# Placing four table columns in the route and the others in the layer's head, in a kernel of linear attention and two expert layers

## The chip, the cores and the metric

The kernel runs on one core of one Trainium2 chip. The metric is the device time of the whole program in microseconds. An execution of the kernel before takes 586.45 us in the median of three (585.61 to 586.54). One more was profiled; the times of the trace are microseconds from the start of its span.

## What is computed

Attention writes 3072 rows of 384 numbers. Each of two expert layers then finds the best of 8 experts for every row, and multiplies the row by that expert's two weight matrices (384 x 1024 and 1024 x 384). In the first layer a row is left alone where its skip score is not positive; in the second every row is replaced.

```python
def _moe_ref(x, w_skip, w_gate, w1, w2) -> np.ndarray:
    ...
    logits = xc @ w_gate
    e_idx = np.argmax(logits, axis=1)
    ...
    gate_w = probs[np.arange(len(xc)), e_idx]
    y = np.zeros_like(xc)
    for e in range(E):
        mask = e_idx == e
        ...
        h = np.maximum(xc[mask] @ w1[e], 0.0)
        y[mask] = gate_w[mask, None] * (h @ w2[e])
    out[do_compute] = xc + y
```

## The kernel before

Three blocks run one after another for each layer's boundary: `attention`, then for each layer m (0 and 1; layer one and layer two in the text) `route` and `moe`. Each is a block of five engine programs with its own semaphores, and between blocks all engines meet at a barrier. Inside a block each engine goes through its own queue in the order in which it is written.

`route` sorts the 3072 rows (24 chunks of 128, `TILES`) by expert. In layer two it first loads the rows back, turns them on PE, copies them out on ACT and DVE (`x_out`, L567) and computes the logits. In both layers DVE then runs a chain of some twenty small operations: best expert, softmax sum (`den`, whose reciprocal is the gate), ranks, and for each row a slot of a table. The slot has a row of the table (`row_i`, slot mod 128) and a column (`col_i`, slot / 128). The table has 128 rows and 38 columns in layer one, 45 in layer two (`NCOL`); column t holds the row ids, and the gates, of the 128 rows that tile t of the expert work takes.

The table is filled on PE. For each chunk, `row_hot` (128 x 128, is the slot's row equal to this one) is the stationary side, and `col_hot` (128 x 2 NCOL: one-hot column times the id, one-hot column times the gate) the moving side; 24 products add up in PSUM (L688). They are float32 products; each stands in the trace as two instructions. DVE makes the column comparison (L781), the gates' half (L784) and `row_hot` (L572, eight operations); ACT makes the ids' half (L721, 24 operations). At the end DVE copies the sums into `table` (L802, L803). Between these stand pieces of another job: the weights of the first expert are split into a high part (`w_hi`, ACT, L856) and a low part (`w_lo`, DVE, L861), fourteen pieces of each, six for w1 and eight for w2. `stay_warm` (L22) runs transposes on PE that nobody reads.

`moe` begins with a head: Pool gathers the first rows (two tiles in layer one, four in layer two) by the table's first columns (L1038), PE turns them (`turn_x`, L1115), ACT rounds them to the high part (`x_high`, L1203), DVE subtracts for the low part (`x_low`, L1252). In the head PE first runs four transposes (L1121) and 24 warm-up transposes (L22). Then come the experts, in units of tiles: `up` (L1132 to L1134, eight column blocks k, each of nine float32r products; block k >= 4 waits for `h_lo` of block k - 4, made by ACT and DVE, L1220, L1221, L1292), then `down` with the second matrix, whose results DVE multiplies by the gate (L1269) and Pool scatters (L1059). While a unit runs, ACT and DVE split the next expert's weights. At the end of layer one SP waits for the last scatter and loads the rows for layer two's route (`load_rows`, L455, L457), in groups of 512 rows.

In layer two's route the programs of ACT and DVE stand inside a loop of one turn whose first instruction is put at the start of a line of instructions (`from_line_start`, `head_slot` 0), so that entering it is a jump.

## Time and profile before

| | us |
|---|---|
| median of three executions | 586.45 |
| the profiled execution, whole | 586.31 |
| its span (first to last instruction) | 584.3 |
| PE busy, matmul | 545.2 |
| DVE busy | 381.5 |
| ACT busy | 262.8 |
| Pool busy | 250.0 |

The mean granted clock of PE over the span is 0.977 of full speed. A reader should look at where layers begin. Attention ends at about 133, layer one's route runs from 133 to 151 and its experts from 160 to 290. Layer two's rows are loaded from 296, its route ends at 337, and its experts run from 347 to 577. Since PE is nearly always busy in between, the timeline of the short stretches around the two routes says more than the page's totals.

### The profile page before, as it was taken

How to read it: one execution, taken by the hardware profiler on the slowest of the kernel's cores; microseconds unless marked ns; L12 is line 12 of the kernel's file. 1: busy time of each engine (PE TensorE's matmuls, PEld its weight loads, DVE VectorE, ACT ScalarE, POOL GpSimd, SP SyncE). 2: the span in 40 equal slices, each digit the busy share in tenths (PEclk: the TensorE clock that was granted, in tenths of full speed). 3: DMA queues.
4: the chain of work that ended last, by engine and by line, in shares of the span. 5: the costliest groups of instructions: out<-in, count | busy, mean ns of one | idle time of the engine just before them, and what ended most of it. 6: DMA issues, size and time to landing. Idle time of an engine off the chain costs nothing. (4 is left out here: it accounts for less than half of the span.)

```text
span 584.3 us, 16263 instructions
## 1 busy us (share of the span) xinstructions
PE 545.2 (93%) x5606; PEld 517.6 (89%) x5607; DVE 381.5 (65%) x832; ACT 262.8 (45%) x752; POOL 250.0 (43%) x356
## 2 busy tenths in 40 slices
PE   4899999988699999999969869999999999999994
PEld 4799999978699999999967859999999999999994
DVE  5789888958598888888704917463747463637341
ACT  1233333325477667776504416262737361627230
POOL 5987778732244444555410042232424322425241
PEclk9999999997799999999999989999999999999998
DMA  9788888776287777776378023544354444111101
GB/s 156 135 166 176 163 165 164 153 257 218 56 304 228 214 222 252 243 235 209 65 249 308 1 61 97 196 139 168 116 191 154 158 140 154 50 42 46 41 2 39
DMA packets 114145, 89.59 MB, mean 153 GB/s; under 512 B 80689, under 2 KB 104948, under 8 KB 114097
## 3 DMA queue, kind: packets, MB, share of 16 engines
q1 hardware_dynamic: 105760, 73.96, 44.6%
q0 software_dynamic: 7776, 14.82, 9.2%
q8 instruction: 26, 0.43, 0.3%
q10 hardware_dynamic: 560, 0.20, 0.2%
q14 instruction: 23, 0.18, 0.1%
HBM read 80.44 MB, written 13.27 MB: 160 GB/s over the span
## 5 line engine op out<-in xcount | busy, mean ns | idle before, releaser
L861 DVE TENSOR_TENSOR w_lo<-w_raw,w_hi 128x384 fp32r<-128x384 f32 (+1 forms) x224 | 130.1, 607 | 5.6 <-ACT w_hi L856 3.4
L1132 PE MATMUL e_ps_h<-e_x_hi,w_hi 128*128 128x192 f32 (+3 forms) x384 | 120.8, 315 | 2.6 <-DVE e_x_lo L1252 2.6
L856 ACT CAST w_hi<-w_raw 128x384 fp32r<-128x384 f32 (+1 forms) x224 | 120.0, 566 | 4.0 <-issue 4.0
L1133 PE MATMUL e_ps_h<-e_x_lo,w_hi 128*128 128x192 f32 (+3 forms) x384 | 120.6, 314 | 0.0
L1134 PE MATMUL e_ps_h<-e_x_hi,w_lo 128*128 128x192 f32 (+3 forms) x384 | 120.5, 314 | 0.0
L1292 DVE SCALAR_TENSOR_TENSOR e_h_lo<-e_ps_h,e_h_hi 128x128 fp32r<-128x128 f32 (+1 forms) x192 | 70.2, 395 | 46.6 <-ACT e_h_hi L1221 43.1
L1132 PE MATMUL e_ps_y<-w_hi,e_h_hi 128*128 128x384 f32 x272 | 95.5, 351 | 0.0
L1134 PE MATMUL e_ps_y<-w_hi,e_h_lo 128*128 128x384 f32 x272 | 91.5, 336 | 0.0
L1133 PE MATMUL e_ps_y<-w_lo,e_h_hi 128*128 128x384 f32 x272 | 91.1, 335 | 0.0
L1132 PEld LDWEIGHTS e_ps_h<-e_x_hi,w_hi 128*128 128x128 f32 x384 | 73.7, 192 | 4.9 <-DVE e_x_lo L1252 3.1
L1133 PEld LDWEIGHTS e_ps_h<-e_x_lo,w_hi 128*128 128x128 f32 x384 | 73.7, 192 | 1.3
L1134 PEld LDWEIGHTS e_ps_h<-e_x_hi,w_lo 128*128 128x128 f32 x384 | 73.6, 192 | 1.3
L1220 ACT ACTIVATE e_h_lo<-e_ps_h 128x64 fp32r<-128x64 f32 x128 | 29.3, 229 | 79.1 <-PE e_ps_h L1134 76.0
L1221 ACT ACTIVATE e_h_hi<-e_ps_h 128x256 fp32r<-128x256 f32 (+1 forms) x128 | 59.4, 464 | 0.0
L1252 DVE TENSOR_TENSOR e_x_lo<-e_ps_x,e_x_hi 128x384 fp32r<-128x384 f32 (+1 forms) x54 | 28.2, 523 | 45.0 <-ACT e_x_hi L1203 44.7
L1133 PEld LDWEIGHTS e_ps_y<-w_lo,e_h_hi 128*128 128x128 f32 x272 | 51.3, 189 | 0.1
L1132 PEld LDWEIGHTS e_ps_y<-w_hi,e_h_hi 128*128 128x128 f32 x272 | 51.2, 188 | 0.1
L1134 PEld LDWEIGHTS e_ps_y<-w_hi,e_h_lo 128*128 128x128 f32 x272 | 51.0, 188 | 0.0
L1203 ACT CAST e_x_hi<-e_ps_x 128x384 fp32r<-128x384 f32 (+1 forms) x54 | 24.5, 456 | 54.8 <-PE e_ps_x L1115 54.8
L1047 POOL DMA_INDIRECT x_in<-x_rows,e_ent_in x33 | 37.5, 1138 | 26.8 <-POOL e_ent_in L1043 26.8
L1059 POOL DMA_INDIRECT out_dram<-y_rows,e_ent_out x19 | 18.5, 973 | 62.7 <-DVE y_rows L1269 54.6
L224 ACT COPY xT<-ps_x 128x384 f32<-128x384 f32 x24 | 11.5, 480 | 71.4 <-PE ps_x L368 71.4
(170 smaller groups left out, 932.8 us busy)
## 6 DMA issues: line engine op xcount, KB each, us to landing
w_raw<-in_moe_w_dram SPq DMA_DIRECT2D x32, 1536.0 KB, 7.0
r_in<-in_r_dram SPq DMA_DIRECT2D x24, 192.0 KB, 3.2
k_in<-in_k_dram SPq DMA_DIRECT2D x24, 192.0 KB, 4.1
v_in<-in_v_dram SPq DMA_DIRECT2D x24, 192.0 KB, 4.0
x_rows<-rows SPq DMA_DIRECT2D x24, 192.0 KB, 3.4
w_lo<-x_rows SPq DMA_DIRECT2D x5, 768.0 KB, 9.4
w_lo<-x_rows SPq DMA_DIRECT2D x2, 384.0 KB, 3.6
x_in<-x_rows,e_ent_in POOLq DMA_INDIRECT x33, 3.1
```

Of the source, the lines that this page charges most:

```text
L856: act.copy(self._of(self.hi1[par], self.hi2[par], n), self._of(self.raw1[par], self.raw2[par], n)).then_inc(self.hi_done[par], 1)
L861: eng.tensor_tensor(self._of(self.lo1[par], self.lo2[par], n), self._of(self.raw1[par], self.raw2[par], n), self._of(self.hi1[par], self.h ...
L1047: pool.indirect_dma_start(x_in[n][:], None, rows, bass.IndirectOffsetOnAxis(ap=ent_in[n][:, 0:1], axis=0), bounds_check=bound, oob_is_err= ...
L1059: pool.indirect_dma_start(out_rows, bass.IndirectOffsetOnAxis(ap=ent_out[slot][0:count, 0:1], axis=0), y_rows[slot][0:count, :], None, bou ...
L1132: pe.matmul(o, s_hi, m_hi, start=(k == 0), stop=False)
L1133: pe.matmul(o, s_hi, m_lo, start=False, stop=False)
L1134: return pe.matmul(o, s_lo, m_hi, start=False, stop=(k == last))
L1203: act.copy(x_hi[:, :, w], ps_x[n % 2][:, 0:D].rearrange("p (c t) -> p c t", c=DC)[:, :, 0:w.stop - w.start]).then_inc(x_hi_done, 1)
L1220: act.activation(h_lo[:, k, top_at:top_at + HALF], ps_h[k % 4][:, TOP], ACT.Relu).then_inc(h_top_done, 1)
L1221: act.activation(h_hi[:, k, :], ps_h[k % 4][:, 0:XW], ACT.Relu).then_inc(h_hi_done, 1)
L1252: dve.tensor_tensor(x_lo[:, :, w], ps_x[n % 2][:, 0:D].rearrange("p (c t) -> p c t", c=DC)[:, :, 0:w.stop - w.start], x_hi[:, :, w].bitcas ...
L1292: ins = dve.scalar_tensor_tensor(h_lo[:, k, lo_at[n]:lo_at[n] + of.stop - of.start], ps_h[k % 4][:, of], 0.0, h_hi[:, k, of].bitcast(F32), ...
```

## The change

In the route only four columns of the table (`AHEAD`) are placed, ids only. The id is split into the number of its 128 rows (`chunk_of`) and its place in them (`part_of`), both small whole numbers, so that float32r products, in one pass, hold them exactly; DVE puts them together. `row_hot` is float32r. Comparisons for all columns, the gates' half (DVE), the ids' half (ACT, twelve operations for the first twelve chunks, DVE for the others) and the 24 float32 products of all columns move into the head of `moe`, on all engines there, with the turns of the first rows between the products. DVE then waits for all 24 (`rest_placed`) and copies the rest of the table and the gates; in layer one eight of the fourteen w_lo pieces come after this. Before, six came after the last `x_low`. The head's 24 warm-up transposes go. ACT has all fourteen w_hi pieces of layer one in the route. The loop that begins a line is taken off ACT's and DVE's programs in layer two's route; a loop of one turn with one register move, at the start of a line, is put at the end of their programs in layer one's `moe`.

```diff
-NOWHERE = 1 << 20
+NOWHERE = 32 * P
+AHEAD = 4
...
+            pool.iota(ids[:], order, base=-NOWHERE, channel_multiplier=1, **exact).then_inc(id_made, 1)
+            pool.iota(chunk_of[:], [[step // P, count] for step, count in order], base=-NOWHERE // P, channel_multiplier=0, **exact).then_inc(id_made, 1)
+            pool.iota(part_of[:], [[0, 1]], base=0, channel_multiplier=1, **exact).then_inc(id_made, 1)
...
             for n in range(PLACES):
-                if n % (PLACES // 2) == 0:
-                    pe.wait_ge(gates_placed, 2 * n // PLACES + 1)
-                pe.wait_ge(ids_placed, n + 1)
+                if n == 0:
+                    pe.wait_ge(few_ready, 2)
                 pe.wait_ge(rows_ready, n + 1)
                 for q in range(GP):
                     i = GP * n + q
-                    ins = pe.matmul(ps_placed, row_hot[:, i, :], placing[:, 2 * NCOL * i:2 * NCOL * (i + 1)], start=(i == 0), stop=(i == TILES - 1))
+                    ins = pe.matmul(ps_few, row_hot[:, i, :], few_hot[:, i, :], start=(i == 0), stop=(i == TILES - 1))
...
-            with from_line_start(act):
...
-                    for n in range(W.N1):
-                        W.hi(act, 0, 0, n)
-                act.wait_ge(id_made, 1)
-                for place in range(PLACES):
...
-                        ins = act.mul(col_hot[:, i, 0, :], col_is[:, i, :], entry[:, i, 0:1])
-                    ins.then_inc(ids_placed, 1)
-                if not TURN:
-                    for n in range(W.N1, W.N):
-                        W.hi(act, 0, 0, n)
+            if not TURN:
+                for n in range(W.N):
+                    W.hi(act, 0, 0, n)
...
-                for n in range(2):
...
-                    dve.tensor_tensor(col_is[:, i, :], row_iota[:, 0:NCOL].unsqueeze(1).to_broadcast(wide),
-                                      col_i[:, i].unsqueeze(2).to_broadcast(wide), ALU.is_equal).then_inc(col_equal, 1)
...
-                    dve.tensor_tensor(col_hot[:, i, 1, :], col_is[:, i, :], entry[:, i, 1].unsqueeze(2).to_broadcast(wide), ALU.mult).then_inc(gates_placed, 1)
...
+            few = [P, TILES, AHEAD]
+            link(dve.tensor_tensor(few_is[:], row_iota[:, 0:AHEAD].unsqueeze(1).to_broadcast(few), col_i[:].unsqueeze(2).to_broadcast(few), ALU.is_equal))
+            dve.wait_ge(id_made, 3)
+            dve.tensor_tensor(few_hot[:, :, 0:AHEAD], few_is[:], chunk_of[:].unsqueeze(2).to_broadcast(few), ALU.mult).then_inc(few_ready, 1)
+            dve.tensor_scalar(few_hot[:, :, AHEAD:2 * AHEAD], few_is[:], part_of[:], None, ALU.mult).then_inc(few_ready, 1)
...
+            link(dve.tensor_scalar(few_at[:], ps_few[:, 0:AHEAD], float(P), float(NOWHERE), ALU.mult, ALU.add))
+            dve.tensor_tensor(table[:, 0:AHEAD], few_at[:], ps_few[:, AHEAD:2 * AHEAD], ALU.add)
...
+        def fetch_next_line(eng):
+
+            reached = eng.alloc_register(f"{tag}_reached")
+            with nc.Fori(0, 1, engines=[eng.engine], head_slot={eng.engine: 0}) as _:
+                eng.reg_mov(reached, 1)
...
+            pool.wait_ge(rest_out, 2)
...
-            stay_warm(pe, ident, ps_y[0][:, 0:P], 3)
-            for n in range(X):
-                turn_x(0, n)
+
+
+            def place(i):
+
+                if i < PART:
+                    pe.wait_ge(gates_hot, 1)
+                    pe.wait_ge(ids_hot, i // 3 + 1)
+                else:
+                    pe.wait_ge(rest_hot, 6)
+                pe.matmul(ps_y[1][:, 0:2 * USED], row_hot[:, i, :].bitcast(F32), hot_of(i), start=(i == 0), stop=(i == TILES - 1)).then_inc(rest_placed, 1)
+            ahead = [PART, PART + 2, PART + 6, PART + 10] if m else [PART, PART + 4]
+            for i in range(TILES):
+                if i in ahead:
+                    turn_x(0, ahead.index(i))
+                place(i)
...
+            act.wait_ge(col_equal, 1)
+            for i in range(PART):
+                ins = act.mul(col_hot[0][:, i, 0, :], is_col[:, i, :].bitcast(F32), ids[:, i:i + 1])
...
+            for n in range(2):
+                i = slice(PART * n, PART * n + PART)
+                wide = [P, PART, USED]
+                dve.tensor_tensor(is_col[:, i, :], row_iota[:, 0:USED].unsqueeze(1).to_broadcast(wide), col_i[:, i].unsqueeze(2).to_broadcast(wide), ALU.is_equal).then_inc(col_equal, 1)
...
+            dve.wait_ge(col_equal, 2)
+            hot(0, 1, gate).then_inc(gates_hot, 1)
+            for n in range(1, 4):
+                hot(n, 0, ids).then_inc(rest_hot, 1)
+                hot(n, 1, gate).then_inc(rest_hot, 1)
...
-                for n in range(W.N1 // 2, W.N1 + 2):
+                for n in range(W.N1 // 2, W.N1):
                     W.lo(dve, 0, 0, n)
             for n in range(X):
                 x_low(0, n)
+            dve.wait_ge(rest_placed, TILES)
+            dve.tensor_scalar(table[:, AHEAD:USED], ps_y[1][:, AHEAD:USED], float(NOWHERE), None, ALU.add).then_inc(rest_out, 1)
+            dve.tensor_copy(gates[:, 0:USED], ps_y[1][:, USED:2 * USED]).then_inc(rest_out, 1)
             if m == 0:
-                for n in range(W.N1 + 2, W.N):
+                for n in range(W.N1, W.N):
                     W.lo(dve, 0, 0, n)
...
             run_experts(dve, expert)
+            if m == 0:
+                fetch_next_line(dve)
```

## Rows read from the trace of the kernel before

**Rows 1.** Busy us by window and engine; then PEclk, DMA share, GB/s

```profile
151.10:157.70 6.60, 4.97 (x24) 5.00 (x25) 2.83 (x5) 0.16 (x1) 2.74 (x2) 0.50 0.15 44
...
160.40:289.80 129.40, 129.39 (x959) 126.92 (x960) 108.91 (x283) 90.64 (x262) 61.21 (x68) 1.00 0.70 223
...
304.70:307.90 3.20, 3.13 (x20) 2.78 (x24) 1.33 (x4) 0.96 (x2) 0.00 (x0) 0.50 1.03 368
...
345.70:352.30 6.60, 5.31 (x17) 5.28 (x17) 1.58 (x3) 1.48 (x4) 2.68 (x5) 0.50 0.16 40
```

**Rows 2.** Timeline of layer one's route: start, us, engine, line, operation, [idle before]

```profile
141.49 0.64 DVE L781 TENSOR_TENSOR m_col_is<-m_row_iota,m_col_i 128x456 f32<-128x456 int32 x1
...
142.23 2.72 ACT L721 ACTIVATE m_placing<-m_col_is,m_entry 128x38 f32<-128x38 f32 x12 [4.49 <-DVE m_col_is L781]
...
142.71 1.96 DVE L572 TENSOR_TENSOR m_row_hot<-m_row_iota,m_row_i 128x384 f32<-128x384 int32 x4
...
143.90 5.48 PE L688 MATMUL m_ps_places<-m_placing,m_row_hot 128*128 128x76 f32 x48
...
147.67 1.89 DVE L861 TENSOR_TENSOR w_lo<-w_raw,w_hi 128x512 fp32r<-128x512 f32 x3
...
147.87 3.39 ACT L856 CAST w_hi<-w_raw 128x384 fp32r<-128x384 f32 x8
...
149.48 0.25 DVE L791 TENSOR_TENSOR m_over_short<-m_seen,m_short_limit 128x96 f32<-128x96 f32 x1
...
150.34 0.19 DVE L802 TENSOR_SCALAR table<-m_ps_places 128x38 int32<-128x38 f32 x1
```

**Rows 3.** Timeline of layer one's head and first unit

```profile
152.73 2.83 DVE L861 TENSOR_TENSOR w_lo<-w_raw,w_hi 128x512 fp32r<-128x512 f32 x5 [2.10 <-issue]
...
153.61 4.84 PE L22 MATMUL e_ps_y<-ident 128*128 128x128 f32 x24
...
154.01 1.52 POOL L1038 DMA_INDIRECT x_in<-x_rows,table  x1 [0.30 <-issue]
...
160.27 2.91 DVE L861 TENSOR_TENSOR w_lo<-w_raw,w_hi 128x384 fp32r<-128x384 f32 x6
...
160.41 0.36 PE L1132 MATMUL e_ps_h<-e_x_hi,w_hi 128*128 128x192 f32 x1 [1.30 <-DVE e_x_lo L1252]
...
163.10 0.48 DVE L1292 SCALAR_TENSOR_TENSOR e_h_lo<-e_ps_h,e_h_hi 128x128 fp32r<-128x128 f32 x2
...
168.58 0.36 PE L1132 MATMUL e_ps_y<-w_hi,e_h_hi 128*128 128x384 f32 x1
```

**Rows 4.** Timeline as layer two begins; landing of the load issued in 296.8:297.3

```profile
303.76 0.86 ACT L567 COPY m_xT<-m_ps_xT 128x384 f32<-128x384 f32 x2 [17.16 <-issue]
...
304.77 2.82 PE L644 MATMUL m_ps_xT<-ident,w_lo 128*128 128x128 f32 x12 [3.56 <-DMA w_lo<-x_rows]
...
w_lo<-x_rows SPq DMA_DIRECT2D x1, 768.0 KB, 7.8
```

**Rows 5.** Timeline of layer two's route and head

```profile
328.13 0.72 DVE L781 TENSOR_TENSOR m_col_is<-m_row_iota,m_col_i 128x540 f32<-128x540 int32 x1
...
334.65 0.35 DVE L795 TENSOR_TENSOR m_over<-m_over,m_of_full 128x192 f32<-128x192 f32 x1
...
336.40 0.20 DVE L802 TENSOR_SCALAR table<-m_ps_places 128x45 int32<-128x45 f32 x1 [0.60 <-PE m_ps_places L688]
...
337.95 0.63 PE L1121 MATMUL e_ps_h<-ident 128*128 128x128 f32 x4 [1.59 <-PEq L482]
...
345.17 0.57 PE L1115 MATMUL e_ps_x<-ident,x_in 128*128 128x128 f32 x3 [0.94 <-DMA x_in<-x_rows,table]
...
347.03 0.68 PE L1132 MATMUL e_ps_h<-e_x_hi,w_hi 128*128 128x384 f32 x1 [1.29 <-DVE e_x_lo L1252]
```

**Rows 6.** The chain of work that ended last, in order of time

```profile
341.91 3.21 DMA x_in<-x_rows,table
...
376.72 0.21 PE e_ps_h L1132
```

More of the change, by code:

```diff
@@ L1 @@
-from contextlib import ExitStack, nullcontext
+from contextlib import ExitStack
 import concourse.bass as bass
@@ L457, in load_rows, with route @@
         eng.dma_start(dst, src).then_inc(x_loaded[g + 1], 16)
-def route(nc, m, W, x_rows, ident, w_g, lg, NCOL, table, starts, order, stored, x_in, x_loaded, fresh_rows):
+def route(nc, m, W, x_rows, ident, w_g, lg, NCOL, table, starts, order, stored, x_in, x_loaded, row_tiles, places):
     tag = f"m{m + 1}"
@@ L480, in route @@
     GW = w_g.shape[2]
+    fresh_rows = row_tiles[1:4] + row_tiles[5:6]
+    row_hot, gate, col_i, ids, row_iota = places
     TURN = m == 1
@@ L566, in x_out @@
                 copy = eng.copy if n == 0 else eng.tensor_copy
[L567 removed]
+                copy(xT[g % 2][b][:], ps_xT[b][:, 0:CH * P]).then_inc(xT_out[n], 1)
         def rows_hot(eng, n):
@@ new lines, in _ @@
+            if TURN:
+                for g in range(TILES // GRP):
+                    x_out(dve, g, 1)
+                dve.wait_ge(l_out, TILES // GRP)
+            link(dve.tensor_reduce(top[:], logits, AX.X, ALU.max))
+            top_all = top[:].unsqueeze(2).to_broadcast([P, TILES, E])
+            dve.tensor_tensor(z[:], logits, top_all, ALU.subtract).then_inc(z_ready, 1)
+            if SK:
+                dve.tensor_scalar(skipped[:], lg[:, :, 0], 0.0, 8.0 * E, ALU.is_le, ALU.mult).then_inc(st, 1)
+                done[0] += 1
@@ new lines, in _ @@
+            dve.wait_ge(ch_ready, 1)
+            dve.wait_ge(exp_done, 1)
+            link(dve.tensor_reduce(den[:], ez[:], AX.X, ALU.add))
+            link(dve.tensor_scalar(den[:], den[:], 1e-9, None, ALU.add))
+            link(dve.reciprocal(gate[:], den[:]))
+            dve.wait_ge(ranked, 1)
+            link(dve.tensor_tensor_scan(seen[:].rearrange("p e i -> p (e i)"), keep[:].rearrange("p e i -> p (e i)"),
+                                        ps_places[:, TILES * E:2 * TILES * E], 0.0, ALU.mult, ALU.add))
@@ new lines, in _ @@
+            count = seen[:, :, TILES - 1:TILES].to_broadcast([P, E, LIMITS])
+            dve.wait_ge(made, 6)
+            dve.wait_ge(limits_made, 3 if m == 0 else 6)
+            link(dve.tensor_tensor(over[:], count, limit[:].unsqueeze(1).to_broadcast([P, E, LIMITS]), ALU.is_gt))
+            link(dve.tensor_reduce(n_tiles[:], over[:], AX.X, ALU.add))
+            link(dve.tensor_tensor_scan(tiles_incl[:], keep[:, 0, 1:1 + E], n_tiles[:], 0.0, ALU.mult, ALU.add))
+            link(dve.tensor_tensor(base[:], tiles_incl[:], n_tiles[:], ALU.subtract))
@@ new lines, in _ @@
+            dve.tensor_scalar(few_hot[:, :, AHEAD:2 * AHEAD], few_is[:], part_of[:], None, ALU.mult).then_inc(few_ready, 1)
+            for place in range(PLACES):
+                rows_hot(dve, place)
+            if not TURN:
+                for n in range(W.N1 // 2):
+                    W.lo(dve, 0, 0, n)
+            if m == 0:
+                link(dve.tensor_tensor(over_short[:], seen[:, :, TILES - 1:TILES].to_broadcast([P, E, MOST]), short_limit[:].unsqueeze(1).to_broadcast([P, E, MOST]), ALU.is_gt))
+                link(dve.tensor_reduce(full[:], over_short[:], AX.X, ALU.add))
+                dve.scalar_tensor_tensor(starts[:, E + 2:2 * E + 2], full[:], float(TALL), base[:], ALU.mult, ALU.add)
+            else:
+                link(dve.tensor_tensor(over[:], over[:], of_full[:].unsqueeze(1).to_broadcast([P, E, LIMITS]), ALU.mult))
+                link(dve.tensor_reduce(full[:], over[:], AX.X, ALU.add))
+                dve.tensor_tensor(starts[:, E + 2:2 * E + 2], base[:], full[:], ALU.add)
@@ L867, in wait_split, with moe @@
         eng.wait_ge(self.lo_done[k][par], (self.N1, self.N - self.N1)[k] * (pair + 1))
-def moe(nc, m, W, rows, out_rows, ident, USED, table, starts, x_in, y_rows, load_next):
+def moe(nc, m, W, rows, out_rows, ident, USED, table, starts, x_in, y_rows, load_next, h_parts, places):
     tag = f"e{m}"
@@ L898, in moe, with hot_of @@
         x_lo = sb("x_lo", [P, DC, XW], F32R)
-        h_hi = sb("h_hi", [P, FC, XW], F32R)
-        h_lo = sb("h_lo", [P, FC, HALF + XW], F32R)
+        h_hi, h_lo = h_parts
+        row_hot, gate, col_i, ids, row_iota = places
+        TILES = gate.shape[1]
+        PART = TILES // 2
+        gates = sb("gates", [P, USED + 4])
+        is_col = h_hi[:].rearrange("p k t -> p (k t)")[:, 0:TILES * USED].rearrange("p (i c) -> p i c", c=USED)
+        col_hot = [sb("col_hot", [P, PART, 2, USED])[:]]
+        FIT = PART // 3
+        col_hot += [y[:, 0:FIT * 2 * USED].rearrange("p (i w c) -> p i w c", w=2, c=USED) for y in y_rows[1:4]]
+        spans_of = [slice(0, PART)] + [slice(PART + FIT * n, PART + FIT * n + FIT) for n in range(3)]
+        def hot_of(i):
+            n = 0 if i < PART else 1 + (i - PART) // FIT
+            return col_hot[n][:, i - spans_of[n].start, :, :].rearrange("p w c -> p (w c)")
         top_at = XW if m else 0
```

188 lines of the change are left out of this document (78 added, 110 removed).

## The prediction

> **What bounds the kernel now.** I read the page's first part, then the stretches by window, then the timeline around the two routes. TensorE (PE) is busy 129.39 of 129.40 us at full clock in layer one's experts [rows 1], so nothing that ACT, DVE, Pool or a load does there shows in the end time. What is left are the gaps at each layer's start: the route, a barrier, and the head in which the first rows are gathered, turned and split. The time moves by what moves the first up-product (160.41 and 347.03 now, [rows 3, 5]), plus whatever PE's clock and PE's waits do just behind it. I cost only these two places, in span time, and add the sum to the profiled execution's own 586.31 us (span 584.3 and 2.0 around it); it lies 0.14 under the median of 586.45.
>
> The clock is the second thing to see. PE is at 0.50 of full speed (1.2 GHz) from 151.1 to 157.7, from 304.7 to 307.9 and from 345.7 to 352.3 [rows 1], each time after a gap in its work, and is back 5.1, 3.2 and 5.4 us after it took up work again (at 152.7, 304.77 and 347.03). In the third stretch 17 up-products take 5.31 us, 0.31 each, where one takes 0.21 at full speed [rows 1, 6]: some 17 x 0.105 = 1.8 us lost on the path. The first stretch costs no up-product anything; it falls on warm-up transposes, 24 in 4.84 us, 0.202 each [rows 3].
>
> **Route of layer one.** DVE sets its length up to the table, ACT its end: ACT's last eight casts end at 147.87 + 3.39 = 151.26, after DVE's table at 150.5 [rows 2]. Out go two comparisons of 0.64 us, two gate products as wide (taken as 0.63), and ACT's 24 products (12 take 2.72 us). In come one comparison and two products of 96 elements, each like the 0.25 of the 96-element row, so 3 x 0.25, and one link more at the table (0.2, the table's own row). The one-hot rows stay, 8 x 0.49 = 3.92 us, three w_lo pieces 1.89, and the small work to the table 0.86 (149.48 to 150.34) [rows 2]. So: 141.49 + 0.7 + 3.9 + 1.9 + 0.85 + 0.35 = 149.2 for the table. ACT, with no products between its casts, is done some 3.4 us after 137.8, long before. PE's products hide: 48 instructions in 5.48 us are 0.114 each, the new ones are 24, so three per 0.49 us of DVE even at that price (a floor of nothing and a ceiling of 24 x 0.114 = 2.7 us, both under DVE's 3.9). The route ends 151.26 - 149.2 = 2.1 us earlier. Two more iotas of Pool lie far ahead of their use.
>
> **Head of layer one.** An engine starts 152.73 - 151.26 = 1.5 us after the last of the route, so at 150.6. What came in: DVE compares twice (1.25), multiplies the first gates (0.65), then six parts (two thirds of 456 elements in all per pair, some 0.3 each, bounds 0.25 and 0.64); ACT makes 12 products in 2.7. PE can place from 152.6. It places 24 tiles in 48 instructions with two turns of three transposes among them, 54 instructions, and the first up-product stands behind all of them on PE's queue. The warm-up of 24 transposes goes. The second gather, issued at 154.01 now and so about 151.9, lands some 3 us later and is not last. At full clock 54 x 0.116 gives 152.6 + 6.3 = 158.9 as the lower end. But PE has done nothing from about 146.5 (the last one-hot row at 142.2 + 3.9, and three placings) to 150.6 and only four transposes till 152.6, more of a gap than that which brought the first stretch at half clock, so I take it to be slow there. Its placing at half clock no row shows: between 0.114 (unchanged) and 0.228 (twice), nearest to the transposes, 0.202. With the clock back 5.1 us after 152.6, 25 instructions are done by 157.7 and 29 x 0.116 = 3.4 follow: 161.1. That is 0.7 us later than 160.41, though the route ended 2.1 earlier. Bounds: 158.9 (never slow) and 161.5 (0.228, back after 5.4).
>
> **The wait that DVE gains.** DVE waits for all 24 placings before it copies the rest of the table and the gates, and behind this wait on its queue stand eight w_lo pieces and then the first h_lo. PE needs the first h_lo before its fifth column block. Now six pieces run from 160.27 and the first h_lo from 163.10 [rows 3]. Then, from the end of placing E: two copies 0.3, eight pieces 8 x 0.485 = 3.9, h_lo 0.48, so E + 4.7. PE's eight blocks take 168.58 - 160.41 = 8.2, so the fifth is reached at E + 4.1: a stall of 0.6. Later blocks come at the same 1.0 us on both engines. Bounds 0 (if E is not when PE starts, but earlier) and 0.9. Layer one: +0.7 + 0.6 = +1.3, bounds -1.5 and +2.0.
>
> **The jump of ACT and DVE.** Now their first copies in layer two's route are at 303.76, with the idle time put down to issue, though PE had turned the first rows by 301.2 (it was idle for 3.56 before 304.77) [rows 4]. It looks like some 3.5 us to win. But PE's next transposes wait for a load issued in the window 296.8 to 297.3 that took 7.8 us to land, so about 304.7, and then go at half clock, 12 in 2.82 us; the copies keep up. I price the jump at nothing; the cover is that load, and were it gone the gain would be up to 304.77 - 301.2 = 3.5.
> The Trainium skill ("Runtime: NRT & Kernel Launch", section on instruction fetch mechanics) says that a taken branch to code outside the fetched pages must first fetch it by DMA. That agrees with ACT's row, and by this rule alone the earlier jump would give the 3.5 us; the row of the load speaks against it.
>
> **Layer two.** Route: from 328.13 on, 0.7 for the three small operations, 3.9, then the six small ones (334.65 to 336.40 less 0.60 of waiting, 1.15), then 0.35: the table at 334.25 for 336.6 [rows 5]. Heads start 337.95 - 336.6 = 1.35 later: 335.6. DVE: 0.72, 0.72 and 0.72 with a wait; PE places from 337.8. It has 48 + 12 instructions, at 0.119 full and 0.207 slow. The gap ahead (from 328.8 + 3.9 + 0.4 = 333.1 to 337.8, but for four transposes of 0.63) makes it slow again; back 5.1 us later, at 342.9, with 25 instructions done, and 35 x 0.119 = 4.2 left: 347.1. The last turn stands two tiles ahead of the end: 346.3. From the last turn to the first up-product now takes 347.03 - 345.17 = 1.86, so the up-product is at 348.1, at full clock. Now it is at 347.03 plus the 1.8 lost behind it, 348.85. Layer two: -0.75. Bounds: never slow, up-product at 346.1, -2.75; the clock back after 5.4 and 0.24 a placing, 0. The last gather is issued at 341.91 now and lands 3.21 later [rows 6], so near 342.8, covered by the placings; if Pool is slower beside DVE by 0.5 us each, still.
>
> **Sum.** +1.3 + 0 - 0.75 = +0.55: 586.31 + 0.55 = 586.9. With the clock back after 3.2 us in both heads it is 152.6 + 3.2 + 38 x 0.116 = 160.2, -0.2 + 0.6, and -1.6 in layer two: -1.2.
>
> **Rivals.**
> 1. PE's clock is back early or never falls in the heads: -1.2 to -0.9 - 2.75 = -3.65. Middle 583.9. For it: one of three rows has 3.2 us, and the placings keep PE busier than the gathers did. Against: two of three rows, and longer gaps ahead of both.
> 2. Slower: the placings stand ahead of the first up-product and are slow. At the 0.228 of a doubled price and with the clock back only after 5.4 us, layer one has E = 161.5, +1.1, and a stall of 0.9, layer two nothing: +2.0, 588.3. It decides from the point at which layer one's first up-product is later than about 161.3. For it: no row has such placings at half clock.
> 3. The jump is what counts (the skill's rule): -3.5 + 0.55, 583.4. It needs the load to land earlier than now.
> 4. The change does not do what it says: the routes are not shorter. Then both heads are 2.1 and 2.4 us later: 591.4. Every operation taken out has its row, so this is small.
>
> **Chances.** Forecast (within 0.2%, 585.3 to 587.6) 0.42; rival 1 0.20; rival 3 0.08; rival 2 0.27; rival 4 0.03. A measurement of this kernel can tell about 0.2%, 1.2 us, from no change. Faster 0.28, same 0.42, slower 0.30. The range that leaves out some 0.1 on each side is 583.5 to 589.0.
>
> **What would show it.** Right: both tables some 2.1 to 2.4 us earlier than now against their route's start; half clock over the placings in both heads; 0.2 us a placing there; layer one's first up-product near 161 and PE idle 0.6 us before its fifth block; ACT's first copy of layer two before 302 and PE still waiting for its load till 304.7; no half-speed up-products in layer two. Wrong: placings at full clock (rival 1), an up-product after 161.5 (rival 2), PE's transposes in layer two's route before 304.

## The result, and the profile after

The changed kernel takes 590.45 us in the median of 20 executions (587.13 to 594.14), the kernel before 586.67 in 20 beside it. The ratio is 1.0069, 95% interval 1.0054 to 1.0085: slower by 0.7%, some 4 us. The forecast was 586.9, and its range ended at 589.0. The profiled execution of the changed kernel took 590.07, with a span of 588.4 where before's was 584.3, so its trace is 4.1 us longer and can be compared with the sum directly. A ratio leaves out executions that took over 1.5% longer than the fastest of the same kernel, which of all the kernels below touches only warm_short, five of its twelve.

The first part of the page of the changed kernel, and the row of the granted clock in 40 slices of 14.7 us:

```profile
PE 551.5 (94%) x5606; PEld 524.5 (89%) x5607; DVE 385.0 (65%) x852; ACT 257.9 (44%) x728; POOL 249.9 (42%) x360
...
PEclk9999999998579999999998969999999999999998
```

PE is busy for 6 us more than in the kernel before (545.2). The slices with 5 and 7 lie at layer one's start. Busy us and count of PE, PEld, DVE, ACT and POOL, then PEclk, DMA share and GB/s, by window, of the changed kernel:

```profile
148.40:152.20 3.80, 1.08 (x4) 0.71 (x4) 2.27 (x10) 1.17 (x6) 1.77 (x2) 0.50 0.06 11
152.20:157.40 5.20, 5.14 (x24) 5.14 (x25) 3.17 (x10) 1.54 (x8) 0.91 (x1) 0.50 0.22 64
157.40:163.60 6.20, 6.20 (x32) 6.20 (x32) 1.11 (x2) 0.96 (x2) 2.62 (x5) 0.50 0.74 281
163.60:168.70 5.10, 5.10 (x26) 5.10 (x26) 4.78 (x13) 1.60 (x6) 1.64 (x1) 0.50 0.06 14
168.90:175.00 6.10, 6.10 (x55) 6.07 (x55) 5.67 (x19) 5.83 (x19) 0.00 (x0) 1.00 0.76 258
333.00:339.40 6.40, 4.51 (x40) 4.33 (x38) 5.18 (x18) 0.00 (x0) 0.00 (x0) 1.00 0.01 3
339.60:349.60 10.00, 8.93 (x42) 8.53 (x42) 4.09 (x10) 3.63 (x14) 5.31 (x6) 0.50 0.27 76
349.80:355.00 5.20, 5.20 (x38) 5.04 (x38) 1.76 (x6) 1.61 (x5) 0.33 (x2) 1.00 0.01 3
```

Most of the result lies here. From 152.2 to 163.6 PE is busy 11.34 of 11.40 us with placings and turns, and its clock stays at 0.50. It comes back only at 168.8, 5.2 us after the first up-product. The kernel before had 6.6 us at half clock there, over transposes that did no work [rows 1]. In layer two the half-clock stretch (6.6 us before, over 16 up-products) is now 10 us long and lies over the placings. The timeline of layer one, changed kernel (start, us, engine, line, operation, idle before):

```profile
142.13 3.83 DVE L566 TENSOR_TENSOR row_hot<-row_iota,m_row_i 128x384 fp32r<-128x384 int32 x8
...
144.20 2.82 PE L683 MATMUL m_ps_places<-m_few_hot,row_hot 128*128 128x8 f32 x24
...
148.73 0.16 DVE L784 TENSOR_TENSOR table<-m_few_at,m_ps_places 128x4 int32<-128x4 f32 x1
...
152.26 5.40 PE L1133 MATMUL e_ps_y<-e_col_hot,row_hot 128*128 128x76 f32 x24 [0.85 <-DVE e_col_hot L1277]
...
158.09 1.83 PE L1133 MATMUL e_ps_y<-y_rows,row_hot 128*128 128x76 f32 x8
...
160.35 3.54 PE L1133 MATMUL e_ps_y<-y_rows,row_hot 128*128 128x76 f32 x16
...
163.63 0.51 PE L1146 MATMUL e_ps_h<-e_x_hi,w_hi 128*128 128x192 f32 x1
...
163.92 0.19 DVE L1296 TENSOR_SCALAR table<-e_ps_y 128x34 int32<-128x34 f32 x1 [2.26 <-PE e_ps_y L1133]
...
164.14 3.83 DVE L842 TENSOR_TENSOR w_lo<-w_raw,w_hi 128x384 fp32r<-128x384 f32 x8
```

The table is made 1.6 us earlier (148.73 for 150.34 [rows 2]), and the first up-product is 3.2 us later (163.63 for 160.41 [rows 3]). The 48 placings run at 0.225 each, in three parts. The same of layer two:

```profile
304.86 0.48 ACT L561 COPY rows<-m_ps_xT 128x384 f32<-128x384 f32 x1 [13.01 <-PE m_ps_xT L640]
...
309.26 2.82 PE L640 MATMUL m_ps_xT<-ident,w_lo 128*128 128x128 f32 x12 [3.02 <-DMA w_lo<-x_rows]
...
338.13 0.16 DVE L784 TENSOR_TENSOR table<-m_few_at,m_ps_places 128x4 int32<-128x4 f32 x1
...
341.69 5.43 PE L1133 MATMUL e_ps_y<-e_col_hot,h_lo 128*128 128x90 f32 x24 [1.07 <-DVE e_col_hot L1277]
...
347.55 1.00 PE L1133 MATMUL e_ps_y<-y_rows,h_lo 128*128 128x90 f32 x4
...
352.32 0.44 PE L1146 MATMUL e_ps_h<-e_x_hi,w_hi 128*128 128x384 f32 x1
```

With the same marks in both traces the 4.1 us divide so. "First comparison" is L781 before and L762 after, the table L802 and L784; the last row of DVE in layer one is at 290.33 before and 295.55 after.

| stretch | before, us | after, us | difference |
|---|---|---|---|
| route one, first comparison to table | 8.85 | 7.24 | -1.6 |
| table to first up-product, layer one | 10.07 | 14.90 | +4.8 |
| first up-product to layer one's last DVE row | 129.92 | 131.92 | +2.0 |
| from there to route two's first comparison | 37.80 | 36.93 | -0.9 |
| route two, first comparison to table | 8.27 | 5.65 | -2.6 |
| table to first up-product, layer two | 10.63 | 14.19 | +3.6 |
| from there to the end of the span | 237.27 | 236.08 | -1.2 |

The routes are shorter, as the diff says, by 4.2 together. The heads are longer by 8.4, and some 24 up-products of layer one now run at 0.215 where they take 0.111. The last row is a gain of about 2.7 (no half-clock up-products in layer two), less a stop of PE at 526.5 to 528.0 that was not there before. The waits of PE after 355, its row in the timeline, and the instruction queue in the DMA view of 520 to 532, all of the changed kernel:

```profile
PE e_ps_h L1146 <- issue: 1.5, 1, 1.5
...
528.02 0.34 PE L1146 MATMUL e_ps_h<-e_x_hi,w_hi 128*128 128x384 f32 x1 [1.47 <-issue]
...
q8 instruction: 2, 0.03, 1.2%
```

PE waits for no engine there, and two packets of instructions are fetched in that window.

### The profile page after: what moved, and what is told of

Its sections match the earlier page's. It is cut to its first block and busy times, and to the rows that moved or that the text cites. A ratio compares the mean times of both kernels' runs of the same rounds, so it can differ in the third digit from the quotient of the medians.

```text
span 588.4 us, 16259 instructions
## 1 busy us (share of the span) xinstructions
PE 551.5 (94%) x5606; PEld 524.5 (89%) x5607; DVE 385.0 (65%) x852; ACT 257.9 (44%) x728; POOL 249.9 (42%) x360
## 5 line engine op out<-in xcount | busy, mean ns | idle before, releaser
L1330 DVE SCALAR_TENSOR_TENSOR h_lo<-e_ps_h,h_hi 128x128 fp32r<-128x128 f32 (+1 forms) x192 | 70.5, 397 | 45.2 <-ACT h_hi L1240 40.6
L1146 PE MATMUL e_ps_y<-w_hi,h_hi 128*128 128x384 f32 x272 | 95.8, 352 | 0.0
L1148 PE MATMUL e_ps_y<-w_hi,h_lo 128*128 128x384 f32 x272 | 91.6, 337 | 0.0
L1147 PE MATMUL e_ps_y<-w_lo,h_hi 128*128 128x384 f32 x272 | 91.5, 336 | 0.0
L1239 ACT ACTIVATE h_lo<-e_ps_h 128x64 fp32r<-128x64 f32 x128 | 29.0, 226 | 80.1 <-PE e_ps_h L1148 78.6
L1240 ACT ACTIVATE h_hi<-e_ps_h 128x256 fp32r<-128x256 f32 (+1 forms) x128 | 59.3, 464 | 0.7 <-issue 0.7
L1147 PEld LDWEIGHTS e_ps_y<-w_lo,h_hi 128*128 128x128 f32 x272 | 51.4, 189 | 0.0
L1146 PEld LDWEIGHTS e_ps_y<-w_hi,h_hi 128*128 128x128 f32 x272 | 51.3, 189 | 0.1
L1148 PEld LDWEIGHTS e_ps_y<-w_hi,h_lo 128*128 128x128 f32 x272 | 51.2, 188 | 0.0
L1217 ACT CAST e_x_hi<-e_ps_x 128x384 fp32r<-128x384 f32 (+1 forms) x54 | 24.5, 454 | 51.4 <-PE e_ps_x L1117 51.4
```

Of the source, the lines that this page charges most:

```text
L1146: pe.matmul(o, s_hi, m_hi, start=(k == 0), stop=False)
L1147: pe.matmul(o, s_hi, m_lo, start=False, stop=False)
L1148: return pe.matmul(o, s_lo, m_hi, start=False, stop=(k == last))
L1217: act.copy(x_hi[:, :, w], ps_x[n % 2][:, 0:D].rearrange("p (c t) -> p c t", c=DC)[:, :, 0:w.stop - w.start]).then_inc(x_hi_done, 1)
L1239: act.activation(h_lo[:, k, top_at:top_at + HALF], ps_h[k % 4][:, TOP], ACT.Relu).then_inc(h_top_done, 1)
L1240: act.activation(h_hi[:, k, :], ps_h[k % 4][:, 0:XW], ACT.Relu).then_inc(h_hi_done, 1)
```

## The experiments

Theory 1: the time is PE's clock. The change takes away the warm-up transposes, and the placings in their stead don't bring the clock back. Against it stood, in turn: the placings cost what they cost, as instructions ahead of the first up-product, at any clock; DVE's new wait; the jump, which may help or harm; and the place of the code in memory, which the change shifts. Each kernel was timed with executions of the kernel before beside it, and ratios are against those.

**warm_gap.** The changed kernel with 16 transposes behind the route's placings and 8 behind the head's first four.

```diff
@@ after the placings in the route
+            stay_warm(pe, ident, ps_xT[0][:, 0:P], 2)
@@ at the head, layer one
+            stay_warm(pe, ident, ps_y[0][:, 0:P], 1)
```

> The changed kernel with 16 transposes that nobody reads after the route's placings (PE has nothing from 147.0 to 150.3 there) and 8 after the head's first four (PE has nothing from 151.4 to 152.3). Theory 1 (the clock: PE falls to half clock in the gap around the barrier, and placings do not bring it back): the heads' placings run at 0.115 instead of 0.225 each, layer one's first up-product comes near 159 instead of 163.6, no up-product is at half clock; 6 to 8 us less than the changed kernel, 582 to 585. Theory 2 (the order: 54 instructions ahead of the first up-product and DVE's pieces behind the wait, whatever the clock): the extra transposes change nothing or cost up to 2 us, 590 to 592.

579.66, ratio 0.9868 (0.9845 to 0.9892). Windows, then the timeline:

```profile
151.20:159.40 8.20, 7.65 (x66) 7.28 (x66) 6.20 (x15) 3.67 (x14) 3.40 (x5) 1.00 0.29 97
...
334.00:341.00 7.00, 5.32 (x46) 5.11 (x47) 3.64 (x10) 3.27 (x13) 4.40 (x5) 1.00 0.32 88
```

```profile
153.19 2.90 PE L1135 MATMUL e_ps_y<-e_col_hot,row_hot 128*128 128x76 f32 x24 [0.47 <-DVE e_col_hot L1279]
...
159.46 0.35 PE L1148 MATMUL e_ps_h<-e_x_hi,w_hi 128*128 128x192 f32 x1
...
159.59 3.83 DVE L843 TENSOR_TENSOR w_lo<-w_raw,w_hi 128x384 fp32r<-128x384 f32 x8
...
163.33 0.49 DVE L1332 SCALAR_TENSOR_TENSOR h_lo<-e_ps_h,h_hi 128x128 fp32r<-128x128 f32 x2
...
163.87 0.36 PE L1148 MATMUL e_ps_h<-e_x_hi,w_hi 128*128 128x192 f32 x1 [0.15 <-DVE h_lo L1332]
```

24 transposes added in each layer, and the kernel is 2% faster than the changed one and 1.3% faster than before (1.7% and 1.0% when it was timed once more, as gap_again). The clock is full in both heads, and a placing takes 0.12 in place of 0.225. DVE's wait shows too now: the fifth block starts at 163.87 where the products before it are 0.11 apart and the last is at 163.45, so PE stood for 0.3.

**warm_head.** The 24 transposes put back in the head alone, ahead of the placings.

```diff
+            stay_warm(pe, ident, ps_y[0][:, 0:P], 3)
```

> The changed kernel with the 24 warm-up transposes of the head put back ahead of the placings, where the kernel before had them. Theory 1: the clock is back some 8 us after the head's start as it was in the kernel before, the placings end near 163, but the up-products behind them are at full clock, 2.5 us less in layer one; layer two within 1 us; 587 to 589. Theory 2: 24 x 0.2 = 4.8 us less 0.9 of waiting come on top in each head, 596 to 599.

583.39, ratio 0.9929 (0.9902 to 0.9957): better than expected. The timeline,

```profile
150.51 4.42 PE L23 MATMUL e_ps_y<-ident 128*128 128x128 f32 x24
...
154.78 2.80 PE L1134 MATMUL e_ps_y<-e_col_hot,row_hot 128*128 128x76 f32 x24
```

and its windows:

```profile
149.50:153.70 4.20, 4.07 (x19) 4.10 (x20) 3.99 (x11) 2.71 (x12) 2.16 (x2) 0.50 0.24 70
154.80:157.40 2.60, 2.60 (x26) 2.60 (x25) 0.00 (x0) 0.00 (x0) 0.00 (x0) 1.00 0.55 107
```

The transposes run slowly and put the first placing 2.5 us later than in the changed kernel, but the clock is back before it, and the placings at full speed win more than that. PE has 24 instructions more in each layer, and the kernel is 1.4% faster than the changed one: what the placings cost is their clock, not their count.

**place_twice.** The changed kernel with each placing issued twice (one product more for each, whose result nothing reads; nothing is left out).

```diff
+                pe.matmul(ps_y[0][:, 0:2 * USED], row_hot[:, i, :].bitcast(F32), hot_of(i), start=True, stop=True)
```

> The changed kernel with each placing of the heads made twice, the first time into a buffer that nobody reads. Theory 1: half clock lasts through all 96 placing instructions in layer one, from about 150 to past 170, since placings do not bring the clock back; a placing instruction stays at 0.225; 11 us more in layer one. The assumption of the prediction (the clock is back some 5 us after PE takes up any work): the clock is back by about 158, and the second half of the placings takes 0.115 each.

601.6 in its one execution, 14.7 over the median of before beside it. Windows:

```profile
151.40:173.00 21.60, 21.55 (x102) 21.55 (x103) 4.28 (x11) 2.49 (x10) 5.16 (x7) 0.50 0.31 99
173.10:178.00 4.90, 4.90 (x25) 4.90 (x25) 4.64 (x13) 1.51 (x5) 0.00 (x0) 0.50 0.00 2
178.20:182.00 3.80, 3.80 (x35) 3.80 (x35) 3.36 (x12) 3.53 (x11) 0.00 (x0) 0.96 0.88 283
```

PE works for 21.6 us almost without a pause and stays at half clock the whole time; the clock returns some 5 us after the first up-product, which is at 173.06. Twice the placings did not bring it back sooner than once. In its layer two it did come back before the up-products: at 359.4, 11 us after the first placing there (348.44), while placings and one turn ran. So placings do not keep the clock down for good; what differs between the two layers is not known. The other traces with the changed kernel's head (long_body, old_jump, pad_pe) repeat it: half clock over all placings of layer one, and in layer two back before they end.

**before_cold.** The other side: the kernel before without the 24 transposes in its heads.

```diff
-            stay_warm(pe, ident, ps_y[0][:, 0:P], 3)
```

> The kernel before without the 24 warm-up transposes of both heads, which is the one part of the change by itself. Theory 1 says that they brought the clock back in layer one: without them half clock lasts until up-products have run for some us, so that 25 or so of them take 0.215 instead of 0.11 (2.5 us), less up to 1 us by which the first up-product comes earlier; layer two about as before or 1 us worse: 587.5 to 589 where before is 586.3. If they only fill the time: 585.5.

589.6, ratio 1.0043 (1.0017 to 1.007). Windows:

```profile
160.60:165.50 4.90, 4.90 (x23) 4.90 (x24) 3.00 (x8) 1.50 (x5) 2.36 (x3) 0.50 0.98 352
...
350.70:356.60 5.90, 5.87 (x18) 5.87 (x19) 1.22 (x2) 1.17 (x3) 3.27 (x6) 0.50 0.23 68
```

and the first up-product in the timeline:

```profile
160.59 0.53 PE L1131 MATMUL e_ps_h<-e_x_hi,w_hi 128*128 128x192 f32 x1 [2.27 <-issue]
```

Its first up-product is where it was (160.59), though the last low part that it needs is there at 159.43: for the 1.2 us between, PE waits for nothing that the trace shows. Then 23 up-products run at half clock, and layer one's later part is 2.4 us longer. The trace is 3.7 us longer in all; 1.1 of it lies between the layers, where nothing was removed. So the transposes that seemed to cost nothing, and whose removal I priced at nothing, were worth 0.4% even with no placings in the head.

**before_warm.** The kernel before with six transposes between the gather turns of layer two's head.

```diff
+                if m and n < X - 1:
+                    for _ in range(6):
+                        pe.transpose(ps_y[0][:, 0:P], ident[:], ident[:])
```

> The kernel before with six more transposes that nobody reads between the four turns of layer two's head, where PE waits 0.7 to 0.9 us for each gather and the clock fell at 345.7. If half clock cost the up-products what the rows say (17 at 0.32 instead of 0.17): 2.5 us less than before, 584. It also tells what the change of the placings is worth with the clock held in both: the changed kernel with its gaps filled took 579.7; if this one takes 584, some 4 us. If the clock in layer two's head does not matter: 586.5.

583.76, ratio 0.9961 (0.9943 to 0.998). From the first up-product of layer two to the last of DVE's rows 226.60 us in place of 229.35: the half-clock up-products of layer two cost 2.75, where I had worked out 1.8.

**warm_route and warm_short.** Each half of warm_gap alone: the 16 behind the route's placings, or the 8 in the head.

```diff
@@ warm_route
+            stay_warm(pe, ident, ps_xT[0][:, 0:P], 2)
@@ warm_short
+            stay_warm(pe, ident, ps_y[0][:, 0:P], 1)
```

> The changed kernel with only the 16 transposes after the route's placings, none in the head. Theory 1, if the gap around the barrier is what lets the clock fall: 580 to 582, as with both. If the second, shorter gap before the first placing is enough to lose it: half clock comes with the placings and stays through them, 586 to 590.

> The changed kernel with only the 8 transposes of the head, none after the route's placings; the mirror of the run with only the 16. If each gap by itself is enough to lose the clock before the placings: half clock in both heads, 588 to 590. If the head's 8 bring it back: at full clock before the placings end, 581 to 584.

warm_route: 588.96, ratio 1.0065 (1.004 to 1.0091). So the 16 alone win nothing. Its windows:

```profile
144.00:147.50 3.50, 3.50 (x34) 3.50 (x33) 3.50 (x8) 0.00 (x0) 0.00 (x0) 1.00 0.00 1
147.60:149.50 1.90, 1.78 (x10) 1.38 (x8) 1.40 (x9) 0.00 (x0) 0.00 (x0) 0.52 0.00 0
...
161.30:165.00 3.70, 3.70 (x35) 3.70 (x34) 2.50 (x7) 1.25 (x4) 2.02 (x4) 1.00 0.40 121
```

Here the clock falls at 147.7, in the middle of the 16 transposes (146.64 to 149.4), though PE has been busy for 3.5 of 3.5 us ahead. What stood there are the route's new placings, 24 of 8 columns in 2.82 us. It would be easy to blame the narrow products, but warm_gap has the same route, and its clock held over the same rows:

```profile
147.70:149.80 2.10, 2.05 (x19) 1.81 (x18) 1.52 (x9) 0.00 (x0) 0.00 (x0) 1.00 0.00 0
```

So it did in gap_again, gap_old_jump and lo_first. Why it fell in this execution stays open. The clock is back at 161.2, 8.4 us after the head's first placing. Layer two of warm_route is the cleaner case:

```profile
336.47 1.97 PE L23 MATMUL m_ps_xT<-ident 128*128 128x128 f32 x16
...
341.84 5.11 PE L1134 MATMUL e_ps_y<-e_col_hot,h_lo 128*128 128x90 f32 x24 [1.53 <-DVE e_col_hot L1278]
```

The 16 transposes run at full clock and it lasts through the barrier; then PE stands for 1.5 us ahead of the first placing, and from 342.1 to 348.9 the clock is at half. That is the gap which the 8 transposes fill. warm_short: the median of all twelve executions is 581.86, and they lie from 576.46 to 588.22. The ratio is 0.99 (0.9864 to 0.9936) with the seven faster ones, and the median of all would stand at 0.992. The profiled one was the longest, with half clock over all of layer one's placings and over the first 1.7 us of layer two's, so whether 8 transposes suffice depends on the execution. The 16 alone never did (588.22 to 593.21 in nine). Both together lie from 578.85 to 581.39 in warm_gap and from 577.97 to 582.45 in gap_again.

**lo_first.** warm_gap, with DVE's eight w_lo pieces ahead of its wait for the placings.

```diff
-            dve.wait_ge(rest_placed, TILES)
-            dve.tensor_scalar(table[:, AHEAD:USED], ...)
-            dve.tensor_copy(gates[:, 0:USED], ...)
...                (the w_lo pieces)
+            dve.wait_ge(rest_placed, TILES)
+            dve.tensor_scalar(table[:, AHEAD:USED], ...)
+            dve.tensor_copy(gates[:, 0:USED], ...)
```

> The changed kernel with both gaps filled, and DVE's eight w_lo pieces moved ahead of its wait for the 24 placings. In the filled kernel PE's matmuls in layer one's first unit stand 0.4 us apart more once, before the fifth block, which I put down to the first h_lo behind these pieces. Expected: the gap is gone, 0.4 us less, 579.2 if 579.7 is without; if DVE's order costs nothing, no change in the trace's gap.

580.51, ratio 0.9917 (0.9885 to 0.995), where warm_gap has 0.9868 and gap_again 0.9902; the intervals overlap. The timeline:

```profile
158.09 3.83 DVE L843 TENSOR_TENSOR w_lo<-w_raw,w_hi 128x384 fp32r<-128x384 f32 x8
...
162.05 0.47 DVE L1332 SCALAR_TENSOR_TENSOR h_lo<-e_ps_h,h_hi 128x128 fp32r<-128x128 f32 x2
```

The first h_lo comes at 162.05, 3.2 after the first up-product at 158.83, where warm_gap had it 3.9 after, and PE no longer stands. A few tenths of a microsecond can't be told in the runs. The wait is real and small.

**old_jump, new_jump, gap_old_jump.** The jump put back to where it was in the changed kernel; the moved jump alone in the kernel before; and warm_gap with the old jump, beside warm_gap once more (gap_again).

```diff
@@ old_jump and gap_old_jump: in the route
+            with from_line_start(act):
...
+            with from_line_start(dve):
@@ new_jump: in the kernel before, layer one's tail
+            if m == 0:
+                fetch_next_line(act)
...
+            if m == 0:
+                fetch_next_line(dve)
```

> The changed kernel with the jump of ACT and DVE back at the start of layer two's route, the rest as changed. If the jump is worth nothing, as predicted, since PE waits for a load: within 0.7 us of the changed kernel, ACT's first copy some 3 us later after the barrier and PE's transposes of the second group at the same distance from the load's issue. If it were worth what it shows: 3.5 us more, 594. If the new place of the code is what made the changed kernel slower (PE's own line fetch of 1.5 us in layer two): up to 1.5 us less.

> The kernel before with only the jump moved: ACT's and DVE's loop at the start of a line goes from layer two's route to the end of layer one's experts. If the load hides it, as predicted: within 0.3 us of before, the time from the load's issue to the first operation of layer two's route (24.5 us in before) unchanged. The kernels with the new jump have 23.7 to 24.3 us there and those with the old one 24.5 to 26.0, so it may be worth 0.5 to 1.5 us: 585 to 585.5 where before is 586. Not 3.5 us.

> The changed kernel with both gaps filled (16 transposes after the route's placings, 8 in the head), once more, beside the next one on the same chip: 0.985 to 0.989 of before, as in its first run.

> The same with the jump of ACT and DVE back in layer two's route. Both have the clock in the heads, so their difference is the jump. If the load hides it always: the same time within 0.5 us. If the first copies are late in part of the executions, as DVE's was in the run with the old jump (310.1, after the load had landed at 309.3): 1 to 2 us more on average, and the time from the load's issue to the route's first operation above 24.5 us. If it is what the run of before with the new jump says (0.5% less): 3 us more.

old_jump: 592.32, ratio 1.0082 (1.0059 to 1.0106), for 1.0069 with the moved jump. new_jump: 583.79, ratio 0.995 (0.992 to 0.9981). gap_again: 580.3, 0.9902 (0.9865 to 0.9939); gap_old_jump 581.42, 0.9914 (0.9882 to 0.9946). All three pairs have the moved jump as the faster, by 0.1 to 0.5%; but only in new_jump does the interval against before lie wholly below 1, so that there is a gain. The timeline of old_jump, and below it that of gap_old_jump:

```profile
309.33 0.55 PE L644 MATMUL m_ps_xT<-ident,w_lo 128*128 128x128 f32 x3 [2.57 <-DMA w_lo<-x_rows]
...
310.14 1.02 DVE L565 COPY x_in<-m_ps_xT 128x384 f32<-128x384 f32 x2 [13.56 <-PE m_ps_xT L644]
...
310.75 2.18 PE L644 MATMUL m_ps_xT<-ident,w_lo 128*128 128x128 f32 x9 [0.88 <-DVE x_in L565]
```

```profile
301.04 0.55 PE L644 MATMUL m_ps_xT<-ident,w_lo 128*128 128x128 f32 x3 [2.35 <-DMA w_lo<-x_rows]
...
301.65 1.02 DVE L565 COPY x_in<-m_ps_xT 128x384 f32<-128x384 f32 x2 [13.37 <-PE m_ps_xT L644]
```

The load still ends PE's wait, but DVE's first copies come 0.6 to 0.8 us after it, and PE, out of buffers, stands 0.9 us more in old_jump (0.7 in gap_old_jump). The cover that I gave the jump is the load, and it is thinner than I took it to be. In before_cold and before_warm, which have the old jump too, PE's second group waits for ACT's copy (4.1 and 3.2 us) and not for the load. From the issue of the load to route two's maximum old_jump takes 26.0 us and the changed kernel 23.8: beside the 0.9 us, the half clock of the transposes lasts till 316.7 there and till 312.2 here. But gap_old_jump takes 24.1 us, and warm_gap 24.3 and gap_again 21.3, which are one kernel; so a difference of 2 us in this stretch can be the execution's.

In new_jump's own trace the copies are early (299.4), yet the same stretch takes as long as before (25.0 for 24.5 us), so its 0.5% is not seen there. It is seen in the clocks of its executions: seven of twelve have a mean clock of 0.978 or more over the span, and take 581.9 us in the mean; the other five, the profiled one (0.974) among them, take 586.5. Of the 35 executions of the kernel before beside it, eight have such a clock (583.6 us; the others 586.8). So the gain lies in executions in which the clock stays up longer. That the jump brings this about is not shown.

**long_body and pad_pe.** For the 1.5 us stop of PE: is it the place of the code? long_body has the route's 64 warm-up transposes as four turns of 16 in place of eight of 8, so all code behind is shifted and nothing else changes. pad_pe was to shift it by 24 register moves.

```diff
@@ long_body
-            stay_warm(pe, ident, ps_xT[0][:, 0:P], 8)
+            with pe.Fori(0, 4) as _:
+                for _ in range(16):
+                    pe.transpose(ps_xT[0][:, 0:P], ident[:], ident[:])
@@ pad_pe
+            pad = pe.alloc_register(f"{tag}_pad")
+            for n in range(24):
+                pe.reg_mov(pad, n)
```

> The changed kernel with the route's 64 warm-up transposes written as 4 turns of 16 instead of 8 turns of 8: the same work, more instructions in PE's program ahead of the layers. The clock in the heads as in the changed kernel. If the place of the code makes PE's stop of 1.5 us in layer two: the stop is gone or elsewhere, 1 to 1.5 us less than the changed kernel. If it is not the place: the stop stays at the same matmul.

> The changed kernel with 24 register moves on PE at the end of each route, no work on the array: the clock stays as in the changed kernel, half through the placings. The changed kernel's PE stands still for 1.5 us at 526.5 in layer two with nothing to wait for, and one line of instructions is fetched there; the filled kernels, with as many more instructions on PE, have no such stop. If the place of the code makes it: the stop goes or moves under other work, up to 1.5 us less, 589. If not: it stays, 590.5.

pad_pe: 589.91, ratio 1.0071 (1.0045 to 1.0097). The moves left no instruction in PE's program (both traces have 16259 instructions), so it is the changed kernel once more, with the same stop (1.48 us). long_body: 588.28, ratio 1.0041 (1.0019 to 1.0063). The window in which the changed kernel stood:

```profile
526.00:534.00 8.00, 8.00 (x48) 7.92 (x48) 4.84 (x9) 4.96 (x13) 3.61 (x6) 1.00 0.21 61
```

PE is busy throughout, and layer two's later part is 1.7 us shorter (226.40 for 228.10), with the clock in both heads as in the changed kernel. So the stop comes with the place of the code. The other traces agree: it is in the three whose PE program is the changed kernel's own (1.47 us there, 1.48 in pad_pe, 1.90 in old_jump), and in none of the nine, long_body among them, in which that program was altered. That PE stands there for a fetch of instructions fits the two packets, but is not shown. By the trace it is worth 1.5 to 1.7 of the 4 us; the ratios (1.0041 for 1.0069) fit that, though their intervals overlap.

## Why the prediction was wrong, step by step

**The step that failed: "with the clock back 5.1 us after 152.6".** I had three rows in which the clock came back 5.1, 3.2 and 5.4 us after PE took up work, and took "work" to be any. In all three PE did transposes of 128 columns or up-products. Over placings it came back late (8.0 us after the first one in layer two, 8.4 in warm_route, 11 in place_twice's layer two) or not at all: not in the 11.4 us of the changed kernel's layer one, not in the 21.6 of place_twice's. It cost 163.63 for 161.1 at the first up-product, and some 24 up-products at half speed behind it that the sum didn't have (2.5 by their spacing). Layer one came to some +5.2 in place of +1.3, over the bound of +2.0. The bound was wrong for the same reason: both of its ends had the clock back before the placings end.

**The same step in layer two.** The clock was back 11.4 us after the end of the table's operation (338.29), where I had 342.9 - 334.25 = 8.7. Two errors of the other sign hid that. The last turn stands 0.9 us ahead of the first up-product (351.42 and 352.32), not the 1.86 that I carried over from [rows 5], so from the same end to the up-product it is 14.03 for 13.85. And the gain behind was mis-sized: up-products without the half clock gave 2.75, not 1.8, since I had compared 0.31 with 0.21, the price of a wider product, and these take 0.173 (at half clock 0.32, and there were 16 of them). But for PE's stop, layer two is -2.6 + 3.6 - 2.75 = -1.8, better than the -0.75 of the sum.

**The sum against the trace.** Of the 3.5 us between +0.55 and +4.1, layer one has 3.9, the way into layer two -0.9, layer two -1.0, PE's stop 1.5.

**The price of a placing** at half clock was 0.225, not 0.202; of the two neighbours it was the bound of twice the full price that held.

**The removal of the warm-up** stood in the working at no price. before_cold shows that it is a loss by itself, 0.4%, and warm_head that putting them back wins 1.2 to 1.4% over the changed kernel. A transpose whose output nobody reads was on no one's path, and the clock it held was on PE's.

**Right in the main:** route one (table done at 148.89, forecast 149.2), the head's start (150.32 for 150.6), the first placing (152.26 for 152.6), and route two (-2.6 for -2.35 at the table). How DVE's wait acts is right as well: the stall of 0.6 is there as 0.3 once PE is at full clock (warm_gap); in the changed kernel it is none, because PE's first blocks, at half clock, come slower than DVE's work.

**The jump.** ACT's first copy is at 304.86 and the load ends PE's wait at 309.26: hidden, as forecast. But with the jump where it was, DVE's copies are behind the load by 0.6 to 0.8 us in two traces, so the jump is not worth nothing: 0.9 us of standing in old_jump, and up to 2.2 with the half clock that lasts longer there. The runs of that pair put it at 0.1%. The 0.5% of new_jump goes with a clock that stayed up in more of its executions; why stays open.
The Trainium skill ("Runtime: NRT & Kernel Launch", section on instruction fetch mechanics) has a taken branch to code outside the fetched pages wait for a fetch. That fits what the first copies do: with the jump alone moved they come at 299.4 in place of 303.76 [rows 4]. Of the 3.5 us that I worked out by that rule, the load kept most from the end time in the traces. The pair of old_jump and the changed kernel leaves 3.5 out; new_jump's interval (0.992 to 0.9981) does not.

**Not foreseen:** PE's stop of 1.5 us, in no rival. long_body and the traces with an unaltered PE program tie it to the place of the code.

**The rivals.** Rival 2 had the right sign and cause, placings that are slow ahead of the first up-product, and the right point of decision (later than 161.3). Its size was 2.0 in place of 4 because it, too, gave the clock back after 5.4 us. Rival 1 was the opposite of what happened, yet warm_gap is that case made true by 24 transposes a layer: it took 579.66 where rival 1 had 583.9. Its trace is 5.6 us shorter than before's, where rival 1 had 3.65 at best: layer one has -1.5 for -0.9, layer two -4.4 for -2.75, which was mis-sized as above. Rivals 3 and 4 fell.

**What the change is worth** with the clock held: warm_gap stands at 0.9868 and 0.9902 of before, and the kernel before with its own half clock in layer two mended (before_warm) at 0.9961. Some 0.6 to 0.9%, 3.5 to 5.5 us, is left for shorter routes and the jump together. By warm_gap's trace it is less: the routes are 4.2 us shorter, but the heads are still 1.7 longer (10.29 and 12.12 us from table to first up-product), so some 2.5 us; the rest of its gain, 3.3 us behind layer two's first up-product, is mostly what before_warm has too. The version that beats both kernels is the changed one with the two groups of transposes, at about 580.

## What to carry to other kernels

Before small products are moved into a place where PE has just stood idle, ask at which clock they will run and what has brought the clock back there so far; a row at full clock prices them only if something keeps it. Work that looks idle (warm-up transposes) is taken out last and alone. A shortened stretch ahead of a barrier is worth its length only if the gap behind it is filled at both ends: 16 transposes ahead and 8 behind did it; the 16 alone did not, and the 8 alone in part of the executions.

## What the runs showed of the hardware

- A half clock that a gap has left may outlast work that keeps PE full by its records: 11.4 us, most of it f32 products of 76 columns at 0.225 each, in layer one of the changed kernel, and 21.6 in place_twice. In layer two it ended over such products, after 8.0 and 11 us. The 24 transposes of warm_head brought it back before they were done. Yet products of the same kind hold a full clock once it is there (24 in 2.90 in warm_gap). The Trainium skill ("TensorE: Matmul & The Clock Gate", the part on the clock gate) says that the clock follows how busy PE has lately been; read from the busy times of the records, layer one's rows say otherwise, and they decide here.
- The same code can keep or lose the clock: over the same 24 products of 8 columns and 16 transposes it fell at 147.7 in warm_route, with PE busy 3.50 of 3.50 us ahead, and held in four other traces (PEclk 1.00 in warm_gap from 147.7 to 149.8).
- PE stood for 1.47 us in the middle of a stream of products, waiting for nothing, with two packets of instructions fetched around it; it was there in three traces of the same PE program (1.47, 1.48 and 1.90) and gone in nine with another. The Trainium skill ("Runtime: NRT & Kernel Launch", section on instruction fetch mechanics) has the cost of streaming code as mostly hidden. If this stop is such a fetch, which no trace shows, it is one that was not.
- With the clock near such an edge, the spread of a kernel grows: warm_short 576.46 to 588.22, for 578.85 to 581.39 in warm_gap and 577.97 to 582.45 in gap_again.
